# First eight q and k pairs: 2 KB rows from DRAM, turned by 64x64 identity products instead of full transposes

## What is computed

```python
# q, k, v: (8 batches, 8 heads, 576 tokens, 64), chunks of 64 tokens
scores = scale * q_c @ k_c.T ; scores -= scores.max(-1)
attn   = exp(scores) / (sum(exp(scores)) + 1e-9)
x      = (attn @ v_c), heads side by side          # (4608, 512)
x      = x / sqrt(mean(x*x) + 1e-6) * rms_g
x      = (silu(x @ w_gate) * (x @ w_val)) @ w_out   # 512 -> 1536 -> 512
h      = x @ w_in ; out = (h * clip(h + 3, 0, 6) / 6) @ w_out2   # 512 -> 2048 -> 512
```

## Time and profile before

| | us |
|---|---|
| median of 3 runs | 1664.08 |
| lowest, highest | 1663.04, 1668.9 |
| profiled execution, its own time | 1670.3 |
| its span in the profile | 1668.5 |
| PE busy | 1626.0 (97%) |
| DVE, ACT, POOL busy | 1034.4, 866.7, 726.2 |

### The profile page before, as it was taken

The page is one execution under the profiler, slowest core; times in us unless marked ns, Lnnn a source line. Parts: engine busy times, 40 slices in busy tenths (PEclk is TensorE's granted clock), DMA queues, the critical chain, the costliest instruction groups (busy, mean ns, idle before and its releaser), DMA issues.

```text
span 1668.5 us, 31535 instructions
## 1 busy us (share of the span) xinstructions
PE 1626.0 (97%) x12297; PEld 1583.9 (95%) x12297; DVE 1034.4 (62%) x1407; ACT 866.7 (52%) x1375; POOL 726.2 (44%) x686
## 2 busy tenths in 40 slices
PE   7889999999999999999999999999999999999999
PEld 5678898999999999999999999999999999999999
DVE  5877778868755556555544776665666864444443
ACT  4665666655544445544444665554665653433432
POOL 2543433449776664322120376777676510010010
PEclk9999999999999999999999999999999999999999
DMA  9676676644565555989997856647648976666664
GB/s 179 140 188 151 165 188 168 162 148 141 186 226 193 201 207 182 341 302 315 312 312 285 302 212 230 225 176 254 220 176 304 383 239 208 197 220 208 197 220 133
DMA packets 334692, 366.98 MB, mean 220 GB/s; under 512 B 185104, under 2 KB 300560, under 8 KB 331344
## 3 DMA queue, kind: packets, MB, share of 16 engines
q1 hardware_dynamic: 322976, 334.69, 63.6%
q0 software_dynamic: 7104, 28.84, 4.8%
q10 hardware_dynamic: 4464, 1.44, 0.5%
HBM read 200.80 MB, written 164.10 MB: 219 GB/s over the span
## 4 chain that ended last, share of the span: by engine, by line
PE 82%; DVE 4%; issue 3%; DMA 3%; POOL 3%; SPq 3%; ACT 2%; DVEq 0%; ACTq 0%; POOLq 0%
PE bx L934 12%; PE by L934 12%; PE bx L936 12%; PE bx L935 12%; PE by L935 12%; PE by L936 12%; PE att L934 2%; PE att L936 2%; PE att L935 2%; DMA hl_b<-h_scratch 2%; DVE tx L1454 1%; SPq L539 1%; PE att L909 1%; PE att L900 1%; PE att L858 1%
## 5 line engine op out<-in xcount | busy, mean ns | idle before, releaser
L934 PE MATMUL bx<-tx,wr 128*128 128x384 f32 x840 | 288.1, 343 | 3.4 <-ACT gb L1130 2.0
L934 PE MATMUL by<-tx,wr 128*128 128x384 f32 x840 | 288.2, 343 | 1.3 <-DVE ub L1479 0.8
L936 PE MATMUL by<-tx,wr 128*128 128x384 f32 x840 | 281.9, 336 | 0.0
L935 PE MATMUL by<-tx,wr 128*128 128x384 f32 x840 | 281.8, 336 | 0.0
L936 PE MATMUL bx<-tx,wr 128*128 128x384 f32 x840 | 281.7, 335 | 0.0
L935 PE MATMUL bx<-tx,wr 128*128 128x384 f32 x840 | 281.5, 335 | 0.0
L1505 DVE TENSOR_TENSOR hl_d<-hl_d 128x1536 fp32r<-128x1536 f32 x84 | 148.4, 1797 | 120.2 <-ACT hl_d L1210 120.2
L1505 DVE TENSOR_TENSOR hl_b<-hl_b 128x1152 fp32r<-128x1152 f32 x84 | 115.1, 1380 | 116.7 <-ACT hl_b L1210 115.8
L1210 ACT ACTIVATE hl_d<-hl_d 128x1536 fp32r<-128x1536 f32 x84 | 122.6, 1482 | 99.6 <-DMA hl_d<-u_scratch 99.6
L934 PEld LDWEIGHTS bx<-tx,wr 128*128 128x128 f32 x840 | 158.4, 189 | 8.6 <-issue 3.5
L934 PEld LDWEIGHTS by<-tx,wr 128*128 128x128 f32 x840 | 158.5, 189 | 6.1 <-DVE ub L1479 2.0
(11 more groups left out here) (184 smaller groups left out, 4248.6 us busy)
## 6 DMA issues: line engine op xcount, KB each, us to landing
hl_d<-u_scratch SPq DMA_DIRECT2D x84, 768.0 KB, 4.5
hl_b<-h_scratch SPq DMA_DIRECT2D x84, 576.0 KB, 6.3
u_scratch<-ut SPq DMA_DIRECT2D x48, 576.0 KB, 3.7
h_scratch<-ht SPq DMA_DIRECT2D x36, 576.0 KB, 3.6
u_scratch<-ub SPq DMA_DIRECT2D x96, 192.0 KB, 2.8
u_scratch<-ub SPq DMA_DIRECT2D x48, 384.0 KB, 2.5
h_scratch<-vb SPq DMA_DIRECT2D x72, 192.0 KB, 3.3
h_scratch<-vb SPq DMA_DIRECT2D x36, 384.0 KB, 3.1
```

What stands on the lines that cost most here:

```text
L934: pe.matmul(dst, w_hi, m_hi, start=start, stop=False, skip_group_check=not opens)
L935: pe.matmul(dst, w_hi, m_lo, start=False, stop=False, skip_group_check=not opens)
L936: return pe.matmul(dst, w_lo, m_hi, start=False, stop=stop, skip_group_check=not opens)
```

## The change

q and k of pairs 0 to 7 are fetched for two pairs at once. The destination is now `[P, NQ // 2, 2, 2, D]`: for two pairs (four batches), for q or k, for even or odd heads `e`. A partition holds a group of eight tokens of one head: 16 (batch, head of that parity) x 8 groups are the 128 partitions, and each is one run of 8 tokens x 64 = 2 KB in DRAM. A transfer is 256 KB in 128 pieces. SP issues 12 of these instead of 24 transfers of 128 KB, ACT 4 instead of 8; the order of q, k, v and the weights stays about the same.

A pair's half of the partitions (64) now holds, for each of the eight token places `r` in a group, a 64x64 block. `turn_qk` turns each of these with a plain matmul with the data as weights and the identity as moving operand: 8 x 2 = 16 for q and 16 for k, 64x64x64 each, where there were 4 and 4 transposes of 128x128. PSUM then holds the tokens in the order (r, group), and `copy_q` and `copy_k` read it with a step of 64 elements to write `qkT` in token order.

```diff
-        def load_first(n, src, which, loaded):
-            t, p = tp_of(n)
-            for c in range(2):
-                sp.dma_start(qk_first[c * CH:(c + 1) * CH, n, which, :].rearrange("t (h d) -> t h d", d=DH),
-                             src[2 * p + c, :, t * CH:(t + 1) * CH, :].rearrange("h t d -> t h d")).then_inc(loaded[n], 16)
+        def load_first(n2, src, which, loaded):
+            for e in range(2):
+                sp.dma_start(qk_first[:, n2, which, e, :], first_of(src, n2, e)).then_inc(loaded[n2], 16)
...
+    def first_of(src, n2, e):
+        t, p = tp_of(2 * n2)
+        return src[2 * p:2 * p + 4, :, t * CH:(t + 1) * CH, :].rearrange("c (j e) (g r) d -> e (c j) g (r d)", e=2, g=TG)[e]
...
-                pe.wait_ge(loaded[n], 32)
-                by_batch = turn_bank(n)[:, i, :].rearrange("p (c j t) -> p j c t", c=2, j=HJ)
-                for j in range(HJ):
-                    tr = pe.transpose(by_batch[:, j], qk_first[:, n, i, j * P:(j + 1) * P], ident[:, :])
+                pe.wait_ge(loaded[n // 2], 32)
+                rows = slice(n % 2 * CH, (n % 2 + 1) * CH)
+                for r in range(CH // TG):
+                    for e in range(2):
+                        tr = pe.matmul(turn_bank(n)[e * CH:(e + 1) * CH, i, r * CH:(r + 1) * CH],
+                                       qk_first[rows, n // 2, i, e, r * DH:(r + 1) * DH], ident[rows, rows], start=True, stop=True)
...
-            act.activation(qkT[:, 1, :], turn_bank(n)[:, 1, :], ACT.Copy).then_inc(k_transposed, 1)
+            act.activation(in_token_order(qkT[:, 1, :]), as_turned(n, 1), ACT.Copy).then_inc(k_transposed, 1)
...
-            dve.tensor_copy(qkT[:, 0, :], turn_bank(n)[:, 0, :]).then_inc(q_transposed, 1)
+            dve.tensor_copy(in_token_order(qkT[:, 0, :]), as_turned(n, 0)).then_inc(q_transposed, 1)
...
+        load_first(0, q, 0, q_loaded_first)
+        load_first(1, q, 0, q_loaded_first)
+        load_first_v(0)
+        load_first(2, q, 0, q_loaded_first)
+        load_first(2, k, 1, k_loaded_first)
+        load_first_v(1)
+        load_raw_a(0)
+        load_first(3, q, 0, q_loaded_first)
+        load_first(3, k, 1, k_loaded_first)
+        load_first_v(2)
+        load_raw_a(1)
```

31 lines of the change are left out of this document (13 added, 18 removed).

## The result

The changed kernel takes 1677.14 us (median, 1675.15 to 1680.97) against 1664.08 for the kernel before in the runs beside it: 1.0077 times as long, 95% interval 1.006 to 1.0093. That is slower by more than 0.5%, and 5 us above the upper end of the forecast range. The profiled execution took 1675.15, with a span of 1673.3.

What follows compares the result with a forecast made beforehand. Only the stretch before the first product (45.8 us) was taken to matter, with the turn on the pass's ring. Gains -7.8, turns +7.7 and POOL's `inverse_rms(3)` +0.3 made +0.2 on 1664.08: 1664.3 us, range 1658 to 1672.

Steps and rivals of the forecast that it cites:

- what a turn costs: Turn of q and k on PE: 64 records, 2.1 us against 1.06, 7.7 us in all after 0.6 hidden.
- The account of places and pace: New turn on PE: two places in the array, each taking a record every 0.06 us, so 32 sets of two.
- The rival of serial records: New turn: column halves sharing rows do not run side by side; 4.0 us a turn, 15 more, 1679; chance 0.09.
- the fast one: New turn: the set of four comes from the queue, not the places; 1.2 us a turn, 1658; chance 0.09.
- the copies: Copies out of PSUM with a step of 64 elements: no change, `copy_k` stays at 0.60 us.
- The rival of stepped reads: Copies out of PSUM: reading with a step costs up to 4.8 us, 1669; chance 0.12.
- the raw weights leave the path: Weight copy on ACT: first raw weights land at about 20 instead of 28.6, ending ACT's wait of 4.76 us.
- the 7.8 us of the sum: Gain ahead of the first product: ACT's wait 4.76, slow clock 1.6, waits for v 1.0, norm's wait 0.4.
- the filler products last until 8, so nothing: First turn: its 1 MB of q and k lands at 6.0 to 7.7, before the fillers end, so no cost.
- My stepping: Loop over pairs: passes stepped one by one, beginning at 14.8, 19.4, 24.1, 28.7, 33.4 and 38.0 us.
- so the array sets this pace and not the issue: Scores on PE: the same work took 1.13 us at the slow clock, so the array limits records; basis for the turn's 2.1.
- PE with no gap at 28 to 33 and the granted clock at 1.00 throughout: Sign expected in the profile after: PE's idle stretch and slow clock gone; the clock's part of the gain was 1.6 us.

Runs made afterwards that it cites:

- the second execution: The changed kernel, unaltered, run and profiled again, against the kernel before: 1678.7 us, ratio 1.0067.
- The wide turn: Changed kernel with the new turn's matmuls twice as wide and half as many (half the turned values zero), against the kernel before: 1671.8 us, ratio 1.0029.
- the first execution: The changed kernel as first profiled, nothing further altered: profiled time 1675.15 us; median 1677.14, ratio 1.0077 to the kernel before.

## Why the prediction was wrong

**Right: what a turn costs.** 64 records, 2.08 us (forecast 2.1), and the pass of 4.64 (4.7). The account of places and pace was borne out further than needed: one column half alone takes a record every 0.067 us. The rival of serial records and the fast one both fall. The Trainium skill, "TensorE: Matmul & The Clock Gate", Part 3, says in its list of what overlaps that a weight load overlaps matmuls under way only where the row group differs. The trace doesn't agree for these matmuls, which share their rows in pairs: 64 loads and 64 matmul records fit in 2.08 us. (The same part also lets a load go ahead that targets the background weight buffer; no run here tells the two apart.) The rows that the prediction showed for this, are a load and its own matmul. The one before is

```profile
46.20 0.33 PE L935 MATMUL bx<-tx,wr 128*128 128x384 f32 x1
```

and the load of L936 begins with it, at 46.20, so the reading stands.

**Right: the copies.** A row of ACT in the regular pass of the changed kernel:

```profile
46.01 0.60 ACT L1079 ACTIVATE qkT<-att 128x512 f32<-128x512 f32 x1 [0.79 <-PE att L886]
```

0.60 us, as before; reading PSUM with a step of 64 elements cost nothing. The rival of stepped reads falls.

**Right: the raw weights leave the path**, and the waits for v with them. L1127 does not wait for the sums. But the size was off: 231 GB/s and not 300 from 8 to 26 us, and a landing at 26.5 (in the run with the transfers alone) in place of 20. I had taken the 2 KB rows as if they ran by themselves at the rate that I read where 512 B and 256 B rows were left; beside v and the others they did not. I had also put nothing for an issue that holds SP. In the changed kernel this cost nothing, as I had worked out for 28.6. It shows with the old turn, where the first product gains 3.2 us and not the 7.8 of the sum (the time 2.7, not clear of noise).

**Wrong: "the filler products last until 8, so nothing".** Two errors in one step. I gave the first MB the whole rate from 2.5 us on. But it shared that rate with what was issued behind it (2.02 MB had moved from 1.5 to 10 us), and the first turn began at 8.5 to 9.7. And the fillers end at 6.95 in the changed kernel, where they had ended at 8.15 before (why the same 12 took less time no run shows). So PE was idle for 2.76 us, with the slow clock at 12 to 15 behind it. My stepping had the first pass begin at 14.8; it began at 18.02, at 15.26 in the second execution.

**Wrong: "so the array sets this pace and not the issue", and with it "PE with no gap at 28 to 33 and the granted clock at 1.00 throughout".** This is the step that decided: the supply of PE's instructions stood in the sum at nothing. In the second execution the passes stand at 15.26 and 19.90, within 0.5 of my 14.8 and 19.4; the third should have begun at 24.1 and began at 29.32. 0.5 us of that came with the start, 3.00 are the block of instructions, the rest is the slow clock behind it. In the first execution the pass that I put at 24.1 began at 29.70, the next at 37.33 in place of 28.7 (its turn took 3.62 us), and from there on the distance to my steps stays at 9: 42.54 for 33.4, 47.18 for 38.0, 54.59 for 45.8. The prediction puts 64 records in place of 8 and prices them by their time in the array alone. None of my rivals had the supply of instructions; the page's q8 queue stood in the profile before, with its 97 packets, and I didn't ask what it would do when a pass needs 272 instructions in 4.64 us in place of 160 in 3.66.

The wide turn shows that this step is what failed. With half the instructions and turns of 1.96 us its passes begin at 14.98, 19.50, 24.02, 28.55, 33.08 and 37.60, where I had stepped 14.8, 19.4, 24.1, 28.7, 33.4 and 38.0, and its first product, forecast for 45.8 + 0.2, comes at 45.01:

```profile
24.02 0.66 PE L895 MATMUL att<-ident,pr 128*128 128x128 f32 x4 [0.75 <-ACT pr L1083]
...
45.01 0.53 PE L948 MATMUL bx<-tx,wr 128*128 128x384 f32 x1
```

So the rest of the sum was right up to the first product, its errors in the transfers notwithstanding. In the first execution of the changed kernel 3.2 us are lost ahead of the first pass (18.02 for 14.8), 2.4 in the pass with the wait (22.66 to 29.70, 7.04 for 4.64), and 3.6 in the two passes behind it at the slow clock (7.63 and 5.21 for 4.64). In the second it is 0.5, 4.8 and 3.7. Here the wait and the slow clock behind it make up nearly all; and the start, once saved, came back as a longer wait.

**What stays open.** By the first product the change should cost 8.7 us; by the medians it costs 12 to 13, with intervals that reach from 8 to 15, so the two need not differ. With the wide turn the first product comes at 45.0 and 46.4, but the median is 6 us above before. The profiled executions show nothing behind the first product that sets the kernels apart (1614.7 to 1622.7 for before, 1618.7 to 1620.7 for the change). It may be that the other executions have more or longer waits for instructions, whose places depend on the traffic; no run shows it.

## What to carry to other kernels

Price a change that trades few large instructions for many small ones twice: by their time on the engine, and by the rate at which they are fetched, which here was about 256 for each 5.4 us while the queues were full. Find it in the profile by gaps "<-issue" in the middle of a group, by the count of records ahead of them, and by the packets of the queue whose kind is instruction. And ask of two gains in one sum whether they end the same wait: here the dearer turn had already used up what the faster transfers had to give, so that the parts alone cost -3.2 and +4.9 us at the first product and together +8.8.

## What the runs showed of the hardware

- PE's instructions come in packets of 16 KB, one for each 127 loads and 127 matmuls; PE stood up to 3.34 us at a border, and went on 1.3 to 1.7 us after the packet's end.
- The issue of a transfer can itself hold its queue: two issues of raw weights took 4.05 us on SP in the changed kernel, 6.05 in the run with the transfers alone, 1.17 before. So in that run the first issue began 8.8 us sooner than before (14.26 for 23.09), and the landing came only 2.1 sooner.
- A change between a 64x64 transpose and a 64x64 two-pass matmul costs about 0.11 us at full clock; 31 of them for each pair, with the slow clock that came with them, made the kernel 62 us slower.
- Two column halves of the same rows run side by side if the matmuls alternate between them (0.031 us a record), and not if they come in a row (0.067).
- A read of PSUM with a step of 64 fp32 elements takes ACT 0.60 us for 512 elements and DVE 0.68, the same as without.
